# Two feed-forward layers behind attention: the widening products computed by Strassen's scheme, on token groups of 768

## What is computed

```python
# x: attention output, (1536, 512)
gate = 1.0 / (1.0 + np.exp(-(x @ w_gate)))      # w_gate, w_val: (512, 1536)
x = (gate * (x @ w_val)) @ w_out                # w_out: (1536, 512)
h = x @ w_in                                    # w_in: (512, 2048)
g = np.where(h >= 1, h, np.where(h <= -1, 0.0, (h + 1) ** 2 / 4))
out = g @ w_out2                                # w_out2: (2048, 512)
```

## Time and profile before

| | |
|---|---|
| runs | 810.24 us median of 3 (810.23 to 810.40) |
| profiled execution | 812.36 us, of which 810.3 us span from the first to the last instruction |
| instructions | 10651 |
| PE, busy | 798.3 us, 4015 matmuls |
| DVE, busy | 377.4 us, 624 instructions |
| ACT, busy | 393.3 us, 636 instructions |
| POOL, busy | 241.6 us, 248 instructions |

### The profile page before, as it was taken

The page is one execution under the profiler, slowest core; times in us unless marked ns, Lnnn a source line. Parts: engine busy times, 40 slices in busy tenths (PEclk is TensorE's granted clock), DMA queues, the critical chain, the costliest instruction groups (busy, mean ns, idle before and its releaser), DMA issues.

```text
span 810.3 us, 10651 instructions
## 1 busy us (share of the span) xinstructions
PE 798.3 (99%) x4015; PEld 687.4 (85%) x4015; DVE 377.4 (47%) x624; ACT 393.3 (49%) x636; POOL 241.6 (30%) x248
## 2 busy tenths in 40 slices
PE   7999999999999999999999999999999999999997
PEld 7899999999888888888888888888888888888886
DVE  5888888888793211131112221234434443344333
ACT  4889988988995332121112232335434333343332
POOL 4567767866865633000000043422100000000000
PEclk9999999999999999999999999999999999999999
DMA  6896586465302331000000023220000100010001
GB/s 140 175 204 139 125 171 140 89 138 122 101 1 74 122 114 55 1 1 1 0 1 1 0 78 105 79 78 27 1 0 1 53 1 0 1 53 0 1 1 52
DMA packets 62002, 49.51 MB, mean 61 GB/s; under 512 B 28592, under 2 KB 51840, under 8 KB 61824
## 3 DMA queue, kind: packets, MB, share of 16 engines
q1 hardware_dynamic: 61792, 48.83, 25.0%
q10 hardware_dynamic: 160, 0.00, 0.0%
HBM read 27.27 MB, written 3.15 MB: 38 GB/s over the span
## 4 chain that ended last, share of the span: by engine, by line
PE 90%; DVE 4%; ACT 3%; issue 2%; DMA 1%; POOL 0%; SPq 0%; ACTq 0%
PE ps L569 17%; PE ps L571 17%; PE ps L570 17%; PE ps L545 6%; PE ps L693 5%; PE ps L695 5%; PE ps L694 5%; PE ps L562 3%; PE ps L563 3%; PE ps L533 3%; PE ps L536 3%; DVE probs L952 2%; PE ps L496 2%; DVE body L963 1%; ACT body L733 1%
## 5 line engine op out<-in xcount | busy, mean ns | idle before, releaser
L569 PE MATMUL ps<-xh,arena 128*128 128x512 f32 x480 | 186.9, 389 | 0.0
L571 PE MATMUL ps<-xh,arena 128*128 128x512 f32 x480 | 186.8, 389 | 0.0
L570 PE MATMUL ps<-xl,arena 128*128 128x512 f32 x480 | 186.8, 389 | 0.0
L425 POOL TENSOR_TENSOR arena<-stage,arena 128x1024 fp32r<-128x1024 f32 (+1 forms) x26 | 73.4, 2831 | 253.5 <-ACT arena L763 253.5
L1022 DVE TENSOR_TENSOR gate<-ps,gate 128x512 f32<-128x512 f32 x36 | 24.9, 692 | 200.6 <-ACT gate L821 200.6
L821 ACT ACTIVATE gate<-ps 128x512 f32<-128x512 f32 x36 | 21.5, 598 | 176.9 <-PE ps L571 176.9
L963 DVE TENSOR_TENSOR body<-ps,body 128x768 fp32r<-128x768 f32 x96 | 91.7, 956 | 32.4 <-ACT body L733 31.2
L569 PEld LDWEIGHTS ps<-xh,arena 128*128 128x128 f32 x480 | 90.1, 188 | 18.9 <-issue 0.4
L571 PEld LDWEIGHTS ps<-xh,arena 128*128 128x128 f32 x480 | 90.1, 188 | 18.8
L570 PEld LDWEIGHTS ps<-xl,arena 128*128 128x128 f32 x480 | 90.1, 188 | 18.6
L418 POOL TENSOR_SCALAR probs<-probs,small 128x768 f32<-128x768 f32 x96 | 86.8, 913 | 25.5 <-DVE small L957 22.7
(11 more groups left out here) (95 smaller groups left out, 1194.0 us busy)
## 6 DMA issues: line engine op xcount, KB each, us to landing
stage<-in_moe_w_out_dram SPq DMA_DIRECT2D x28, 256.0 KB, 3.3
body<-qh SPq DMA_DIRECT2D x15, 384.0 KB, 5.3
body<-kh SPq DMA_DIRECT2D x28, 192.0 KB, 5.4
stage<-in_moe_w_in_dram SPq DMA_DIRECT2D x16, 256.0 KB, 2.8
qn<-in_q_dram SPq DMA_DIRECT2D x16, 192.0 KB, 4.6
kn<-in_k_dram SPq DMA_DIRECT2D x16, 192.0 KB, 5.8
body<-ql SPq DMA_DIRECT2D x16, 192.0 KB, 5.7
vn<-in_v_dram SPq DMA_DIRECT2D x16, 192.0 KB, 2.6
```

The costliest lines, as they stand in the source:

```text
L569: pe.matmul(dst, wh, ah, start=start, stop=False)
L570: pe.matmul(dst, wh, al, start=False, stop=False)
L571: return pe.matmul(dst, wl, ah, start=False, stop=stop)
```

## The change

**Widening by Strassen's scheme (Winograd's form).** A set is one product of the 512-wide activations of one batch (768 tokens) with 256 columns of a weight: gate and value alternate for 2 batches x 6 column pairs in layer one (24 sets), then 2 x 8 sets in layer two. Weight and activations are each cut into 2 x 2 blocks: 256 of the 512 inputs by 128 columns, and 256 inputs by 384 tokens. Instead of eight block products there are seven, each of 2 chunks x 3 matmuls of 384 columns. POOL makes four sums of weight blocks for every set (sums_a, sums_b), and the split is made for seven blocks (round_w on ACT, low_a and low_s on POOL). As the weight sums aren't kept, it is made anew for each batch: 40 times in all. The activations' four sums and the split of seven blocks are made once for each batch and layer, in the last set of the preceding group of sets (sum_x, rest_x on DVE, round_x on ACT); for the first group they are made during attention, some by POOL.

**Reading out.** Product r of set n goes to bank 6 or 7, in turn (4 or 5 in the first two sets), and waits until the product two before it is read out (emptied). ACT copies product 0 to SBUF, DVE adds products 1 to 6 with intermediate sums into the two hidden tiles of 128 x 768, product 4 by two additions. The nonlinear steps then run on hidden tiles in SBUF, of 768 columns, where they ran on PSUM banks of 512 before.

**Narrowing** of a hidden tile follows in units, laid by the function units behind the products of later sets. In layer one a unit is 3 x (512 + 256) columns, and the parts of 256 share two banks, which are zeroed by a matmul with a zero operand at the start of a group; in layer two it is 3 x 512 columns for one of six token blocks. High and low narrowing weights are kept, and made once for each layer.

**The rest.** The SBUF layout is new. The loads are 512 KB each, one for each set (three buffers). The first four products of set 0 stand between the last steps of attention, where two tiles' gate products stood. The output of batch 0 is stored from x during the second group of layer two, that of batch 1 at the end in six blocks.

The core of the diff:

```diff
+    R = 7
+    F = 2 * P
+    N1, N2 = 2 * B * (T1 // 2), B * (T2 // 2)
+    NSETS = N1 + N2
...
+        LEFT = (0, 4, 1, 5, 3, 2, 6)
+        def bank(n, r):
+            q = R * n + r
+            return ps[:, (4 if n < 2 else 6) + q % 2, 0:G]
...
+        def emptied(n, r):
+            if r < 0:
+                n, r = n - 1, r + R
+            return (e_dve, (R - 1) * n + r) if r else (e_act, n + 1)
...
+            def sums_a(n):
+                a11, a12, a21, a22 = blocks(n)
+                pool.wait_ge(raw_in[n % 2], 16 * (n // 2 + 1))
+                if n:
+                    pool.wait_ge(w_split, 2 * n)
+                pool.tensor_tensor(wsum[:, 0], a21, a22, ALU.add).then_inc(sum_parts, 1)
+                pool.tensor_tensor(wsum[:, 2], a11, a21, ALU.subtract)
+                pool.wait_ge(sum_parts, 2 * n + 1)
+                pool.tensor_tensor(wsum[:, 1], wsum[:, 0], a11, ALU.subtract).then_inc(sum_parts, 1)
+            def sums_b(n):
+                pool.wait_ge(sum_parts, 2 * n + 2)
+                pool.tensor_tensor(wsum[:, 3], blocks(n)[1], wsum[:, 1], ALU.subtract).then_inc(w_sums, 1)
+            def low_a(n):
+                pool.wait_ge(w_high, 2 * n - 1)
+                high, low = weights(n, 0), weights(n, 1)
+                pool.tensor_tensor(low[:, 0:2].rearrange("p a c m -> p (a c) m"), raw(n)[:, :, 0:P],
+                                   high[:, 0:2].rearrange("p a c m -> p (a c) m").bitcast(F32), ALU.subtract)
+                pool.tensor_tensor(low[:, 2], blocks(n)[3], high[:, 2].bitcast(F32), ALU.subtract).then_inc(w_split, 1)
+            def low_s(n):
+                pool.wait_ge(w_high, 2 * n)
+                pool.tensor_tensor(weights(n, 1)[:, 3:7], wsum[:, :], weights(n, 0)[:, 3:7].bitcast(F32),
+                                   ALU.subtract).then_inc(w_split, 1)
...
+            for n in range(2, NSETS):
+                sums_a(n)
+                sums_b(n)
+                low_a(n)
+                low_s(n)
+                if n % 2 == 0 and n <= N1 // 2:
+                    f = n // 2 - 1
+                    low_wo(f, f, (narrow(2 * f + 1), narrow(2 * f)))
+                if N1 < n <= FIRSTS[3]:
+                    f = n - 1 - N1
+                    low_wo(T1 // 2 + f, f, (narrow2(2 * f), narrow2(2 * f + 1)))
 
...
+            def product(n, r):
+                if r < 2:
+                    pe.wait_ge(w_split, 2 * n + r + 1)
+                if n in FIRSTS:
+                    pe.wait_ge(x_low, low_count(group_of(n), r))
+                if n == 2 and r == 0:
+                    pe.wait_ge(o_last, 3)
+                if R * n + r > 1:
+                    pe.wait_ge(*emptied(n, r - 2))
+                high, low = weights(n, 0)[:, LEFT[r]], weights(n, 1)[:, LEFT[r]]
+                dst = bank(n, r)
+                for c in range(2):
+                    pe.matmul(dst, high[:, c, :], high_x(r)[:, c, :], start=(c == 0), stop=False)
+                    pe.matmul(dst, high[:, c, :], low_x(r)[:, c, :], start=False, stop=False)
+                    last = pe.matmul(dst, low[:, c, :], high_x(r)[:, c, :], start=False, stop=(c == 1))
+                last.then_inc(p_done, 1)
...
+                for n, (w, h) in enumerate(((wh, hh), (wh, hl), (wl, hh))):
+                    pe.matmul(main, w[:, cols], h[:, t % 3, 0:512], start=(first and n == 0), stop=(last_tile and n == 2))
+                    last = pe.matmul(rest, w[:, cols], h[:, t % 3, 512:S], start=False,
+                                     stop=(last_tile and n == 2 and c % 2 == 1))
...
+            def units(n, r):
+                if n < N1:
+                    return int(n > 1 and (r > 2 if n % 2 == 0 else r < 4))
+                if n == N1:
+                    return (0, 0, 0, 2, 3, 3, 0)[r]
+                if n in (N1 + 1, FIRSTS[3] + 1):
+                    return (0, 0, 0, 0, 2, 3, 3)[r]
+                if n == FIRSTS[3]:
+                    return (2, 2, 1, 2, 3, 3, 3)[r]
+                return (2, 2, 1, 1, 2, 2, 2)[r]
...
+            product(0, 0)
+            product(0, 1)
             turn_probs(STEPS - 3)
             turn_probs(STEPS - 2)
             for part in range(HT):
                 weigh(2 * NH - 2, part)
             turn_probs(STEPS - 1)
+            product(0, 2)
+            product(0, 3)
...
+            def round_w(n):
+                act.wait_ge(raw_in[n % 2], 16 * (n // 2 + 1))
+                if n > 1:
+                    act.wait_ge(p_done, R * (n - 1))
+                high = weights(n, 0)
+                act.copy(high[:, 0:2].rearrange("p a c m -> p (a c) m"), raw(n)[:, :, 0:P])
+                act.copy(high[:, 2], raw(n)[:, 2:4, P:F]).then_inc(w_high, 1)
+                act.wait_ge(w_sums, n + 1)
+                act.copy(high[:, 3:7], wsum[:, :]).then_inc(w_high, 1)
...
+            def value_set(n):
+                g = group_of(n)
+                ahead = n + 1 in FIRSTS
+                first_product(n)
+                if ahead:
+                    round_x(g + 1, 0)
+                    round_x(g + 1, 1)
+                round_w(n + 1)
+                if n < N1 // 2:
+                    f = pair_of(n)
+                    if f == 0:
+                        act.wait_ge(o_ready, 2 * NH)
+                        act.wait_ge(o_done, LATE)
+                    round_wo(f, (narrow(2 * f + 1), narrow(2 * f)))
+                if n == FIRSTS[1] + 1:
+                    empty_y(0)
+                if ahead:
+                    for r in (2, 3, 4):
+                        round_x(g + 1, r)
...
+                if r == 1:
+                    dve.wait_ge(*emptied(n, 0))
+                    if n:
+                        dve.wait_ge(*emptied(n - 1, 6))
+                        if widens(n - 1) == "value":
+                            dve.wait_ge(gated, 2 * pair_of(n - 1) + 2)
+                    dst, other = u2, u1
+                elif r == 2:
+                    if pp > 1 and not value:
+                        dve.wait_ge(hl_ready, 2 * (pp - 1))
+                    dst, other = u1 if value else one[:, 0:G], u1
+                elif r == 3:
+                    dve.wait_ge(*emptied(n, 1))
+                    dst, other = u3, u2
+                elif r == 4:
+                    dve.wait_ge(*emptied(n, 3))
+                    dve.tensor_tensor(two[:, G:S], bank(n, 4), u3, ALU.add)
+                    dst, other = u2, u2
+                elif r == 5:
+                    dst, other = two[:, 0:G], u3
+                else:
+                    dve.wait_ge(*emptied(n, 4))
+                    dst, other = u2 if value else one[:, G:S], u2
+                dve.tensor_tensor(dst, bank(n, r), other, ALU.add).then_inc(e_dve, 1)
...
+            def gate_set(n):
+                t, g = 2 * pair_of(n), group_of(n)
+                empty(n, 1)
+                rest_tile(t - 2)
+                empty(n, 2)
+                if n in FIRSTS:
+                    rest_x(g, 5)
+                    empty(n, 3)
+                    rest_x(g, 6)
+                    rest_tile(t - 1)
+                else:
+                    rest_tile(t - 1)
+                    empty(n, 3)
+                for r in (4, 5, 6):
+                    empty(n, r)
...
+            def value_set(n):
+                g = group_of(n) + 1
+                ahead = n + 1 in FIRSTS
+                empty(n, 1)
+                if ahead:
+                    sum_x(g, 0)
+                    sum_x(g, 1)
+                empty(n, 2)
+                gate_quarter(n)
+                if ahead:
+                    rest_x(g, 0)
+                empty(n, 3)
+                if n == FIRSTS[1] + 1:
+                    empty_y(0)
+                if ahead:
+                    rest_x(g, 1)
+                empty(n, 4)
+                if ahead:
+                    rest_x(g, 2)
+                    rest_x(g, 3)
+                empty(n, 5)
+                if ahead:
+                    sum_x(g, 2)
+                empty(n, 6)
+                if ahead:
+                    sum_x(g, 3)
+                gate_tiles(n)
+                if ahead:
+                    rest_x(g, 4)
...
+            def hinge_set(n):
+                t, g = 2 * pair_of(n), group_of(n)
+                ahead = n + 1 in FIRSTS
+                empty(n, 1)
+                rest_tile(t - 2)
+                if n in FIRSTS:
+                    rest_x(g, 5)
+                if t > TILES1:
+                    add_hinge(t - 1)
+                if ahead:
+                    sum_x(g + 1, 0)
+                    sum_x(g + 1, 1)
+                empty(n, 2)
+                empty(n, 3)
+                if n in FIRSTS:
+                    rest_x(g, 6)
+                rest_tile(t - 1)
+                if ahead:
+                    rest_x(g + 1, 0)
+                    rest_x(g + 1, 1)
+                empty(n, 4)
+                if ahead:
+                    rest_x(g + 1, 2)
+                    rest_x(g + 1, 3)
```

(12 more changed lines are left out.)

815 lines of the change are left out of this document (458 added, 357 removed).

## The result

The changed kernel takes 829.06 us (median of 4 runs, 827.60 to 831.71) beside 810.32 us of the kernel before on the same chip: a ratio of 1.0232, 95% interval 1.0204 to 1.0260. The forecast was 813.6 us with a range of 797 to 828. The direction that had the largest chance (0.46, slower) is right, the size is off by 15.5 us, and the time lies 1 us outside the range. The profiled execution, 831.71 us with a span of 829.6, is the slowest of the four; all that follows is read from it.

The account below looks back on a forecast made before the run. PE was taken as the bound, the feed-forward being a bare stream of matmuls. Terms of -30.4+4.8+3.5+1.5+26.4-2.4 = +3.4 us took the median from 810.24 to 813.6 us, range 797 to 828.

Parts of the forecast that it names:

- The columns: Feed-forward matmuls: fewer columns in widening (gain 33.3 us), first-layer narrowing +2.0, zeroing +0.9; sum -30.4 us.
- rival B: Narrowing: 256-column matmuls take as long as 384-column ones, 0.1745 us each; +15.7 us, 829 us; chance 0.06.
- rival A: Feed-forward: DVE and POOL seldom collide, batch and layer changes cost 12.4 to 20 us; 798 to 807 us; chance 0.31.
- (d): Changes of batch or layer (sets 11/12, 23/24, 24/25, 31/32, 32/33): PE waits for DVE, which POOL delays; +26.4 us.
- POOL's new work in attention ... 0: Last pairs of attention: POOL's 9 us of new work has two steps of slack; 0, up to 2 us without cover.
- The end of attention: Last attention steps and first sets: PE waits for operands, read-outs and ACT; +4.8 us, of it 2.05 at product (0,3).
- Product 6: First-layer value sets: it waits 0.35 us for product 4's read-out by two additions; 10 sets, +3.5 us.
- (c): Steady second-layer sets: no PE waits, DVE's chain for the first tile ends 0.7 us before PE wants it; 0.
- The early pairs: Early first-layer pairs: after gating the next read-out has 0.14 us to spare, which POOL takes; +1.5 us.
- Loads "hidden": Weight loads: half as many, 512 KB each, with two sets to land, so they cost no time.
- C: Read-outs 0.3 us late in each of 7 products in a row without narrowing work: PE loses 10 us, 824; chance 0.12.
- D: Cover holds everywhere: batch and layer changes cost near 3 us, end of attention 2; 785 to 790 us; chance 0.07.

Follow-up runs that it names:

- the kernel with POOL light: Changed kernel with POOL's weight sums and residues made for one column instead of 128 from set 3 on: 812.8 us, ratio 1.0022.
- the kernel with the new order and short instructions: Changed kernel with DVE's next-group sums and residues earlier, narrowing units moved, POOL's residues cut to 256 columns: 831.7 us, ratio 1.0252.

## Why the prediction was right and wrong, point by point

**The columns.** Right. Within a product 384 columns go every 0.175 us, and the step from 256 columns is 0.118 (forecast 0.120), which is against rival B. An early unit of set 14 and the product behind it, after:

```profile
433.83 0.28 PE L760 MATMUL ps<-hh,wo 128*128 128x256 f32 x1
433.94 0.34 PE L729 MATMUL ps<-xop,wset 128*128 128x384 f32 x1
434.12 0.34 PE L730 MATMUL ps<-xop,wset 128*128 128x384 f32 x1
```

What I had too low are small parts of nearly every step, 0.1759 for 384 columns in the place of 0.1745 and 0.2331 and 0.229 for the narrowing's 512, and they make the whole term 5 us smaller. The Trainium skill ("TensorE: Matmul & The Clock Gate", Back-to-back issue gap) would give an estimated 109 ns for 256 columns and a gain 3 us larger; the trace has 118, and the term came out smaller.

**DVE and POOL collide.** The mechanism is shown, against rival A: with one of the two light, 16 to 20 us go, most of it waits, and DVE's residues fall towards 0.95 us. The Trainium skill ("SBUF — State Buffer", Who interferes with whom) has two SBUF inputs hold an exclusive lock and lets a tensor_scalar in two-port mode take it too: this case agrees, the clamp (L1274) takes 0.56 us on the mean in the kernel with POOL light, not the 0.88 I had priced, and 2.34 beside a POOL subtraction of 2.39. After, DVE and POOL:

```profile
658.37 2.34 DVE L1274 TENSOR_SCALAR tmp<-hid 128x768 f32<-128x768 f32 x1
```

```profile
657.91 2.39 POOL L506 TENSOR_TENSOR wset<-wsum,wset 128x1024 fp32r<-128x1024 f32 x1
```

**The failed step is the size of (d).** The prediction says "so I take 8, 7, 5.5, 3.4 and 2.5: +26.4 (bounds 12.4, no collision, and 34)". Measured are 36.9, above the bound, and 0.9 in set 13 beside them. Sets 23/24 came as forecast. At 11/12 (10.8 for 8) and 31/32 (9.0 for 5.5) the meetings cost more than they were priced at: two residues there took 2.84 and 2.01 us in a row for 1.9 us of work, and I took less than the walk gave (8 for 8.5, 5.5 for 6.6). In sets 25 and 33 the forecast had 5.9, and 10.7 were measured. There the walk was about right and a term was left at nothing: the prediction's price for a wait ends with the first matmul behind it (0.165 us), but the matmuls after it ran at the 1.2 GHz level. With the same waits at a full clock the two sets lose 3.6 and 2.8 us, 6.4 in all and close to the forecast; the other 4.3 us are the clock.

**A second failed step: "POOL's new work in attention ... 0".** "Two steps of slack before a transpose wants it" looked at the wrong waiter. POOL's results had slack, but the small sum queued behind each of its new operations had none, and it cost 3.9 us; the price named for the case that the cover is gone, "up to 2 us", was half of it. The stretch in the earlier trace rows had POOL at 165.6 of 242.7 us, but in the last 45 us after the change it is at 39.7, where it was at 31.8 before.

**Smaller terms.** The end of attention: 2.05 forecast at product (0,3), 1.84 measured. Product 6: 0.35 forecast in ten sets, 0.33 measured in each of them (two of the ten stand in the rows of the changes). (c), steady second-layer sets at 0: right, but with little to spare: POOL's last residue for set 30 ended at 644.5 us and product 1 of that set wants it at about 648 (645.8 + 1.05 + 2 x 0.68), which the short instructions used up over the sets. The early pairs' 1.5 us didn't appear. Loads "hidden": right for the time, wrong in the reason, since POOL stood still 35.7 us in all for them and it merely had that time to spare.

**Rivals.** C is refuted as laid: but for product 6, as forecast, no read-out in a run of products is late away from the changes, since PSUM-side operations keep 0.553 us beside POOL. D's premise, that the cover holds, is false for the order that the diff wrote.

**Was it amount or place?** The forecast ends in "Saved columns are spent on waits for DVE", as if the work had to cost that. It hadn't. Taking all of the added work away gives 799.2 us; putting the same work in other places, with POOL's instructions cut shorter, gives 803.4 (805.6 with them whole). DVE's busy time in the feed-forward is 361 us after and 349 in the fastest kernel. Most of the loss was short operations that PE waits for, queued behind long ones that it doesn't. What remains open is how much each single move of the last kernels is worth by itself, as they were run on top of one another, and how much of what they gain together comes from the clock, which falls less often as the waits go.

## What to carry to other kernels

When a change gives idle engines new work, walk each of their queues and ask, for every short operation that another engine waits for, what long one now stands ahead of it; that told more here than busy shares or sums of durations. Two engines' operations on shared memory that meet cost one of them, here, up to the other's length, so price a full stretch by chains of meetings and not by one each, and let the range's end come from that. Count also what a long wait does to the matmuls behind it, wherever PE is the bound again after the wait. Before judging such an idea by its first order, mend the order: one that lost 2.3% gains 0.7 to 1% with the same work in other places.

## What was not expected of the hardware

- A DVE operation with two SBUF inputs of 768 columns took 2.84 us beside POOL's 1024 columns where it takes 0.95 alone; two in a row took 4.8 us. The queued POOL operations didn't starve it: it got in after each.
- Cutting POOL's instructions didn't shorten the total of waits by itself: in the kernel with the new order and short instructions four of 256 columns in a row took 4.99 us beside a busy DVE (at 386.57), 1.25 each, against 0.74 for one free, so POOL pays for the alternation as DVE does.
- After waits of 1.7 to 4 us PE's matmuls ran at the 1.2 GHz level (0.32 us for 384 columns), and the stretches around them show a granted clock of 0.69 to 0.93. Not every such wait brings this: in the run with short POOL instructions the same two waits of set 25, 1.9 and 1.8 us from start to start, left the clock full. Whether it costs anything depends on who is the bound there: nothing at set 12, where product 6 came no earlier at a full clock, but 2.8 us at set 25, where the set took 6.4 us beyond its usual length and 3.6 with the same waits at a full clock.
